# Expert stage of a routed kernel: the DMAs of the first product's way through memory and the weight loads issued by one queue, tile by tile

## The reference

```python
def reference(**kw):
    attn_out = _attn_ref(q, k, v, w_phi)            # 8 x 8 heads, 576 x 64, feature map of 128
    x = attn_out.transpose(0, 2, 1, 3).reshape(4608, 512)
    x = ((x @ w1) * (x @ w2) @ w3) @ w_out          # d_ff 1024
    return _moe2_ref(x, w_gate, moe2_w1, moe2_w2)

def _moe2_ref(x, w_gate, w1, w2):                   # 8 experts: w1 512 x 1024, w2 1024 x 512
    logits = x @ w_gate
    expert_idx = argmax(logits, 1)
    gate_w = softmax(logits)[expert_idx]
    for e in range(8):
        mask = expert_idx == e
        out[mask] = gate_w[mask] * (relu(x[mask] @ w1[e]) @ w2[e])
```

## Time and profile before

| | |
|---|---|
| median of 3 runs | 1525.67 us (1517.71 to 1527.85) |
| profiled execution | 1515.61 us, of which the span from first to last instruction 1513.9 us |
| TensorE busy | 1474.5 us, 97% of the span |
| VectorE, ScalarE, GpSimd busy | 58%, 41%, 36% |
| mean granted clock | 0.993 |

### The profile page before, as it was taken

One profiled execution on the slowest core, in us unless ns is written; L12 is line 12 of the kernel. 1 busy time (PEld: TensorE's weight loads), 2 busy tenths in 40 slices (PEclk: granted clock), 3 DMA queues, 4 the chain that ended last, 5 costly groups with the idle time before them and its releaser, 6 DMA issues.

```text
span 1513.9 us, 29051 instructions
## 1 busy us (share of the span) xinstructions
PE 1474.5 (97%) x8062; PEld 1273.2 (84%) x8063; DVE 881.2 (58%) x1619; ACT 618.4 (41%) x1295; POOL 546.8 (36%) x655
## 2 busy tenths in 40 slices
PE   7999999999999999999999999999999989999996
PEld 6999999999978888888888888887888768888885
DVE  5688888888826374654737465436455444544332
ACT  4688788788812122121222212133344343343221
POOL 5676676676810022020201202113344443343321
PEclk9999999999999999999999999999999999999999
DMA  7354344344430202021120202136677666744441
GB/s 248 119 141 104 107 107 108 102 108 126 107 120 1 70 15 83 0 83 28 55 75 9 83 0 83 28 130 217 214 218 232 220 207 211 230 136 141 142 140 37
DMA packets 111242, 173.49 MB, mean 115 GB/s; under 512 B 52976, under 2 KB 72176, under 8 KB 106978
## 3 DMA queue, kind: packets, MB, share of 16 engines
q1 hardware_dynamic: 76978, 114.01, 25.4%
q10 hardware_dynamic: 26640, 38.81, 8.1%
q0 software_dynamic: 7584, 20.17, 4.4%
HBM read 123.66 MB, written 50.34 MB: 115 GB/s over the span
## 4 chain that ended last, share of the span: by engine, by line
PE 67%; DMA 2%; issue 1%; ACTq 1%; ACT 1%; DVE 0%; POOLq 0%; POOL 0%; DVEq 0%
PE bank L167 65%; PE bank L1690 1%; DMA arena<-rows_scratch,idg 1%; DMA h_scratch<-arena 1%; ACT big L810 0%; ACTq L1248 0%; ACTq L824 0%; PE bank L1621 0%; ACT arena L1228 0%; PE bank L1629 0%; PE bank L1640 0%; POOLq L824 0%; PE bank L1734 0%; PE bank L1615 0%; DVE xs L1448 0%
## 5 line engine op out<-in xcount | busy, mean ns | idle before, releaser
L167 PE MATMUL bank<-big,xs 128*128 (+1 forms) x2100 | 498.1, 396 | 16.6 <-DVE big L610 8.0
L167 PEld LDWEIGHTS bank<-big,xs 128*128 128x128 f32 x2100 | 394.2, 190 | 101.6 <-issue 19.2
L167 PE MATMUL bank<-xs,big 128*128 128x512 f32 x1728 | 397.5, 391 | 2.7 <-PEq L216 2.7
L167 PEld LDWEIGHTS bank<-xs,big 128*128 128x128 f32 x1728 | 324.7, 188 | 70.3 <-issue 2.9
L167 PE MATMUL bank<-big 128*128 128x512 f32 (+1 forms) x1632 | 324.6, 347 | 2.0 <-POOL big L306 1.4
L167 PEld LDWEIGHTS bank<-big 128*128 128x128 f32 (+1 forms) x1632 | 254.6, 164 | 36.2 <-POOL big L306 1.6
L1023 POOL TENSOR_TENSOR arena<-arena 128x512 f32<-128x512 f32 x32 | 40.5, 1277 | 437.4 <-DMA arena<-rec_scratch 437.3
L1417 DVE TENSOR_TENSOR arena<-arena,bank 128x512 f32<-128x512 f32 x72 | 49.5, 687 | 241.6 <-PE bank L167 241.6
L1342 DVE CUSTOM_DVE_ANT_0 arena<-arena 128x512 f32<-128x512 f32 x256 | 159.5, 690 | 17.4 <-ACT arena L1182 17.0
L1162 ACT COPY arena<-bank 128x512 f32<-128x512 f32 x72 | 42.3, 587 | 306.5 <-PE bank L167 306.5
L704 PE MATMUL bank<-arena 128*128 128x66 f32 (+1 forms) x1152 | 147.7, 269 | 0.0
(11 more groups left out here) (180 smaller groups left out, 1361.5 us busy)
## 6 DMA issues: line engine op xcount, KB each, us to landing
arena<-we SPq DMA_DIRECT2D x32, 1024.0 KB, 7.0
h_scratch<-arena ACTq DMA_DIRECT2D x37, 512.0 KB
arena<-h_scratch ACTq DMA_DIRECT2D x148, 128.0 KB
kqraw<-kq SPq DMA_DIRECT2D x32, 576.0 KB, 3.9
rows_scratch<-arena SPq DMA_DIRECT2D x36, 256.5 KB
xT_scratch<-arena SPq DMA_DIRECT2D x32, 288.0 KB
arena<-v SPq DMA_DIRECT2D x64, 128.0 KB, 2.4
arena<-xT_scratch SPq DMA_DIRECT2D x8, 1024.0 KB, 5.4
```

The source lines that it names most:

```text
L167: ins = nc.tensor.matmul(out, left[a], right[b], start=first and n == 0, stop=last and n == 2)
```

## The change

- **SyncE issues the way through memory.** `relu_stored` no longer stores and `load_quarters` leaves ScalarE's loop. SyncE gets a loop over tiles: store the rows of g, then the weight loads of the tile before (`loads_of(g - 1)`), then the four quarter loads of g, after the store has landed and `hq` is free.
- **Weight loads by tile.** A fifth table row, LD, is CH cut off at the last chunk that still has one to load behind it. One counter `w_here` replaces the four: each load waits until all earlier ones have landed.
- **GpSimd**: the ids of the next gather are read and copied ahead of the waits for the kept gate and for TensorE's transposes.
- **Ahead of the loop**: tile 2's relu writes into `hq`, so `h_transpose(1)` can come later; the second product of tile 0 stands directly behind the first product of tile 2, with `x_transpose(3)` after six of its eight steps, and `h_transpose(1)` last.
- VectorE has two more small operations in the table chain, ahead of `tabs`, and a copy of 144 instead of 96 columns.

```diff
-            def load(c, u):
-                sp.dma_start(ahead[:, u * CW:(u + 1) * CW], t["we"][ds(c, 1)].rearrange("a p n -> p (a n)")
-                             ).then_inc(w3_in[u], 16)
...
-            for u in range(3):
-                load(CPE + u, u)
-            for u in range(2):
-                announce(u, 1)
...
-            with sp.Fori(done + 1, NCH // SLOTS) as i:
-                for u in range(SLOTS):
-                    sp.wait_ge(w_lo, SLOTS * i + u - SLOTS + 1)
-                    load(SLOTS * i + u, u)
-                    announce((u + 2) % SLOTS, i - done + (1 if u >= 2 else 0))
+            def load(c):
+                slot = (c % SLOTS) * CW if isinstance(c, int) else sp.snap((c % SLOTS) * CW)
+                sp.wait_ge(w_here, 16 * c)
+                sp.dma_start(ahead[:, ds(slot, CW)], t["we"][ds(c, 1)].rearrange("a p n -> p (a n)")
+                             ).then_inc(w_here, 16)
+
+            def load_into_slot_of(c):
+                sp.wait_ge(w_lo, c + 1)
+                load(c + SLOTS)
+
+            def loads_of(g):
+                first = table(m, sp, LD, g - 1, CPE, NCH - SLOTS)
+                end = table(m, sp, LD, g, CPE, NCH - SLOTS)
+                chunks(sp, first, end, load_into_slot_of)
+
+            def store_rows(g, rows_at):
+                for h in range(2):
+                    sp.wait_ge(relu_done[h], g + 1)
+                sp.dma_start(m["hrows"][ds(g * P, P), :], rows_at).then_inc(h_stored, 16)
+
+            def load_quarters(g):
+
+                sp.wait_ge(h_stored, 16 * g + 16)
+                if not isinstance(g, int):
+                    sp.wait_ge(h_turned, g)
...
+            def tile(g):
+                store_rows(g, hs)
+                loads_of(g - 1)
+                load_quarters(g)
...
             sp.wait_ge(tabs, 2)
-            load(CPE + 3, 3)
...
+            load(CPE + 3)
+            store_rows(2, hq)
+            load_quarters(2)
+            last = tiles(sp, tile)
+            loads_of(last_of(sp, 1))
...
                 else:
                     keep_gate(g - 1)
+                    ids_of(g)
                     pool.wait_ge(gate_saved, g)
+                    pool.wait_ge(xtr_mm, g)
+                gather_rows(g)
...
-                act.wait_ge(relu_done[0], g + 1)
-                act.dma_start(m["hrows"][ds(g * P, P), :], hs).then_inc(h_stored, 16)
...
                 turned_h_high(g - 1)
-                load_quarters(g)
                 tile_chunks(act, g, weights)
...
+            linked(dve.memset(tabf[:, 2, FIRST - 2:FIRST - 1], float(CPE)), base)
             linked(dve.memset(tabf[:, 2, FIRST - 1:FIRST], float(CPE + FIRST - 1)), base)
+            linked(dve.tensor_scalar_min(tabf[:, 4], tabf[:, 2], float(NCH - SLOTS)), base)
...
             ids_by_place()
-            pe.wait_ge(ht_lo, 2)
-            h_transpose(1)
...
             for h in range(2):
                 first_product(2, h, 0, 0)
-            x_transpose(3)
-            second_product(0, 0, 0)
+            second_product(0, 0, 0, between=(6, lambda: x_transpose(3)))
+            h_transpose(1)
```

More of the change, by code:

```diff
@@ L816, in weights_low @@
                             m["ring"][:, 0, ds(at, CW)].bitcast(F32), ALU.subtract).then_inc(done, 1)
-EX, ROW, CH, T = (k * GMAX for k in range(4))
+EX, ROW, CH, T, LD = (k * GMAX for k in range(5))
 def table(m, eng, row, g, least, most):
@@ L843, in stage2 @@
         ids0_in, ids0_set = sem("s2_ids0_in"), sem("s2_ids0_set")
-        w3_in = [sem(f"s3_w_in{i}") for i in range(SLOTS)]
         w_here = sem("s3_w_here")
@@ L986, in _ @@
             turns(sp, turn)
-            def load(c, u):
-                sp.dma_start(ahead[:, u * CW:(u + 1) * CW], t["we"][ds(c, 1)].rearrange("a p n -> p (a n)")
-                             ).then_inc(w3_in[u], 16)
[L992 to L997, removed]
+            def load(c):
[18 more added lines that the diff above has]
+                    sp.wait_ge(h_turned, g)
+                stored = m["hrows"][ds(g * P, P), :].rearrange("(b i) (a c) -> a i b c", i=Q, a=P // Q)
+                for a in range(P // Q):
+                    sp.dma_start(hq[a * Q:(a + 1) * Q, :].rearrange("i (b c) -> i b c", b=P // Q), stored[a]
+                                 ).then_inc(hq_in, 16)
+            def tile(g):
+                store_rows(g, hs)
+                loads_of(g - 1)
+                load_quarters(g)
+            sp.sem_inc(w_here, 16 * CPE)
+            sp.sem_inc(h_stored, 32)
+            sp.sem_inc(hq_in, 128)
             sp.wait_ge(lg_mm, BQ)
@@ L1000, in _ @@
             sp.wait_ge(rows_out, 16 * BQ * NB)
-            for u in range(3):
-                load(CPE + u, u)
-            for u in range(2):
-                announce(u, 1)
+            for c in range(CPE, CPE + 3):
+                load(c)
             sp.wait_ge(w_lo, CPE)
@@ L1050, in keep_gate, with ids_of, gather_rows @@
                 pool.tensor_copy(m["gnext"][:], xg[:, DM:XW]).then_inc(gate_saved, 1)
[L1052 to L1058, removed]
+            def ids_of(g):
                 row = table(m, pool, ROW, g, 0, E * TPE)
                 pool.tensor_copy(m["idg"][:], m["idall"][:, ds(row, 1)]).then_inc(idg_set, 1)
+            def gather_rows(g):
                 pool.wait_ge(idg_set, g + 1)
@@ L1064, in gather @@
                                         ).then_inc(gathered, 16)
+            def gather(g):
+                if isinstance(g, int):
+                    pool.wait_ge(gate_set, g)
+                    pool.wait_ge(xtr_mm, g)
+                    ids_of(g)
+                else:
+                    keep_gate(g - 1)
+                    ids_of(g)
+                    pool.wait_ge(gate_saved, g)
+                    pool.wait_ge(xtr_mm, g)
+                gather_rows(g)
             def scatter(g):
@@ L1219, in relu_half @@
                 act.wait_ge(h_mm, 2 * g + h + 1)
-                if h == 0 and isinstance(g, int) and g > 0:
+                if h == 0 and isinstance(g, int) and g == 1:
                     act.wait_ge(htr_mm, 2 * g)
                 if h == 0 and not isinstance(g, int):
+                    act.wait_ge(htr_mm, 4)
+                if h == 0 and not isinstance(g, int):
                     act.wait_ge(h_stored, 16 * g)
-                out, product = hs[:, h * HF:(h + 1) * HF], h_ps[h][:]
+                out, product = (hq if isinstance(g, int) else hs)[:, h * HF:(h + 1) * HF], h_ps[h][:]
                 if not stored:
@@ L1296, in _ @@
             h_high(1)
-            load_quarters(2)
             act.wait_ge(tabs, 2)
@@ L1708, in second_product @@
                 for j in range(FC):
-                    if j == DC and between is not None:
-                        between()
+                    if between is not None and j == between[0]:
+                        between[1]()
                     if j * DM % CW == 0:
@@ L1774, in _ @@
                 first_product(g, h, *here)
-            second_product(g2, *before2, between=lambda: h_transpose(g))
+            second_product(g2, *before2, between=(DC, lambda: h_transpose(g)))
             last_product(*here)
```

16 lines of the change are left out of this document (3 added, 13 removed).

## The result

The changed kernel takes 1515.57 us (median of 18 runs, 1513.15 to 1517.86) against 1520.22 us of the kernel before in 18 runs beside it (1515.1 to 1527.85): **ratio 0.9961, 95% interval 0.9948 to 0.9975**. The median of before is now 5.5 us under the 1525.67 us from which the prediction started.

What follows compares the result with a forecast made beforehand. TensorE, busy 97% of the span, was taken as the bound, leaving only idle time and lowered clock to win. Middle -12.3 us plus start 0 took 1525.67 to 1513 us, range 1502 to 1527.

Steps and rivals of the forecast that it cites:

- The ring is open; the 12.3 us should go.: Middle: ScalarE's cycle of store, landing, quarters, casts, relu no longer delays turns; all 12.3 us lost there are won.
- I take no loss, bounds 0 and 3 us: SyncE's queue: carrying store, weight loads and quarters in each turn makes no tile late; 0 us, at most 3.
- S: Start of a tile's first product, from which the prediction counts times in a turn of 11.37 us.
- double turn: Turn with two weight loads (tiles 3, 14, 16, 17); quarters issued at S + 16, with 8.5 us to land.
- S + 24.5: Time by which quarters must have landed, as the second product two turns later needs the turned rows.
- rival 3: SyncE's queue: quarters land late behind weight loads, 4.5 us in double turns; 1532 us or over 1541; chance 0.08.
- turns of about 15.5 us: Middle, kernel before: the cycle through ScalarE stretches turns of 11.37 us to about 15.5.
- 0.9 us of slack for VectorE in a turn with two chunks: Middle: with ScalarE freed, TensorE is next late, VectorE having about 0.9 us to spare in such turns.
- Two more small operations add about 0.3 us.: Start: memset and minimum in VectorE's table chain delay the tables by only about 0.3 us.
- The wait is moved.: Start: the wait for gathered rows becomes 4.3 us of idle time for the tables ahead of tile 3; net 0.
- about 4 more: Start: VectorE's table operation ahead of GpSimd's weight operation would gain about 4 us more; left out of the sum.
- That covers the gather's wait.: Middle: earlier casts and gather remove TensorE's 1.24 us wait for the gather, within the 12.3; gather issued within 0.4 us.
- Rival 1: Unprofiled runs have a longer slow stretch, so 3 to 10 us more go: 1503 to 1510 us; chance 0.30.

Runs made afterwards that it cites:

- the best kernels: Changed kernel with quarters between the loads (0.9923), with weights behind tables and table reads ahead too (0.9868), and the latter with TensorE's old order (0.9881).
- the fifth row late: Changed kernel with the fifth table row made behind the tables other engines wait for, SyncE waiting for it by itself: 1511.3 us, 0.9933.
- where the second catch is taken away: Changed kernel with only the second of GpSimd's early weight operations behind the wait for the tables: 1508.3 us, 0.9917.
- both operations out of the way: Changed kernel with GpSimd's two early weight operations behind the second gather and the wait for the tables: 1510.6 us, 0.9938.
- The front order alone: Kernel before with only TensorE's new order ahead of the loop and tile 2's relu in the quarters' buffer: 1520.1 us, 0.9994.
- casts-first kernel: Kernel before with one line moved: ScalarE issues the quarters behind its weight casts instead of ahead of them: 1507.7 us, 0.9912.
- quarters between loads: Changed kernel with the quarters issued behind a turn's first weight load and ahead of a second one: 1508.9 us, 0.9923.

## Why the prediction was right or wrong

The sign and the range held, and 1513 is 2.6 us from the measured time. That is better than the reasons deserve: I forecast a step of -12.3 us, and it was -4.65. The median of before, taken from three runs, was 5.5 us too high and covered for it.

- **"The ring is open; the 12.3 us should go."** The ring was the cause, as one moved line shows (0.9912). But in the changed kernel 6.0 of the 12.3 us stayed. The step that failed is "I take no loss, bounds 0 and 3 us" for what SyncE has to carry. With S at 1188.2 in tile 14's turn, I had put the first load of a double turn 0.2 us behind the store; SyncE's two table reads, which I had put at nothing there, stand between them, and it was 3.45 us. The first load then landed in 4.74 us and not in 7.0, so the first quarter was issued at S + 17.8 instead of S + 16. The last landed 8.6 us later, about the 8.5 that I had in hand, at S + 26.3: 1.8 us behind the S + 24.5 at which I needed them. It is rival 3's mechanism at a third of its price, in the three turns that I had named, and in tile 3's as soon as the start was early. Two readings of mine were off beside it: the "turns of about 15.5 us" were one turn of 15.8, while the eight took 11.4 to 15.8; and the 0.9 us of slack for VectorE in a turn with two chunks wasn't there (48 matmuls in 11.52 us instead of 11.17 at 1194.13, the gathered rows' low half coming only behind a weight operation), which fits the 0.7 us that the best kernels still lose.
- **"Two more small operations add about 0.3 us."** They did, but the chain then ended beside GpSimd's next weight operation, where a copy of 0.2 us takes 5. I had the chain's end at 1050.33, and the same trace has GpSimd's next operation 0.66 us behind it (GpSimd's timeline of the kernel before), which I left out:

```profile
1050.99 4.58 POOL L1105 TENSOR_TENSOR big<-arena,big 128x2048 fp32r<-128x2048 f32 x1
```

  I priced only the case in which the first catch would vanish. The start cost +5.6 us instead of 0. The two operations are not needed for it: with the fifth row late, without them, the copy was caught too.
- **"The wait is moved."** Right, and its size too where the second catch is taken away: 4.39 us of idle time against 4.3 forecast. What I had named and left out of the sum, a table chain that doesn't stand beside GpSimd's weight operation, was worth more than the step itself: with both operations out of the way the start is 5.4 us shorter than before, against "about 4 more".
- **"That covers the gather's wait."** The gather starts 1 us behind the transposes instead of 1.9, not within 0.4; undone, it changes nothing.
- **Rival 1**, a longer loss in the unprofiled runs: these runs do differ by up to 13 us in the kernel before, and the traces speak for it in part. The front order alone leaves the ring as it is, and its profiled execution lost 4.2 us more there than that of before, at 1520.6 us, near the medians of both kernels (1520.1 and 1520.2). And in each of the thirteen kernels with a trace the median's step against before is 1 to 9 us more of a gain than start, turns 3 to 12 and middle give in the profiles (4.65 against 1.1 us for the changed kernel). So the profiled execution of before lost less than is usual, by an estimate from these differences some 4 us. With the 17 us of the front-only kernel in place of its 12.8, the changed kernel's 5.6 us of start and 11 of ring make -5.4, near the measured -4.65. Two more differences between executions are in the traces: the second catch (7 us in the casts-first kernel), and the time of the last matmul of the tables, which ends at 1035.5 to 1041.5 us over the fourteen. How much each has in the spread of before is open.

## What to carry to other kernels

Before a wait and its DMA issues go to another engine, try them later on the same one: the loss was not the issuing but that work which others needed stood behind the wait, and one moved line won more than the new queue as it was first built (middle 3.0 against 6.0 us lost). On the queue that takes them, count every instruction between the old neighbours, table reads too, and put the transfer that is wanted first in front. When a short chain of small operations stretches beside a long one of another engine, as VectorE's did here beside GpSimd's, keep them apart by a wait; a lead of half a microsecond was luck. And set a single profiled execution against the median before summing from it: here one differed from its median by 4.6 us and another by 7.

## What was not expected of the hardware

A VectorE operation is caught although its recorded start is ahead of GpSimd's: 1052.49 against 1052.90 (4.97 us), 1050.59 against 1051.24 (5.24 us), 1053.53 against 1054.18 (5.31 us, casts first). One at 1050.54 against 1051.01 is not (0.23 us, quarters between loads), nor is one at 1050.13 against 1050.99 in the kernel before (0.20 us). The recorded starts don't tell which goes first. The Trainium skill's page "SBUF — State Buffer", section "Who interferes with whom", says that of a VectorE operation and one of GpSimd that need the shared port pair, whichever issues first has it for the whole instruction; the lengths agree (in both pairs shown of the changed kernel VectorE ends within 0.1 us of GpSimd); which one issued first no trace here shows, and the recorded order can't stand for it.
